# Expert rows loaded in blocks and turned by VectorE, gates loaded apart, and the ends of one expert's second layer placed among the first groups of the next

## The reference

```python
def _attn_ref(r, k, v, w, u):              # 2 x 8 heads x 768 tokens x 48
    for t in range(S):
        cur = np.einsum('bhd,bhe->bhde', u[None] * kt, vt)
        y[:, :, t] = np.einsum('bhd,bhde->bhe', rt, state + cur)
        state = w[None, :, :, None] * state + np.einsum('bhd,bhe->bhde', kt, vt)

def _moe_ref(x, w_in, w_out):              # 1536 x 384, hidden 2048
    h = x @ w_in
    g = np.where(h > 0.0, h, np.exp(np.minimum(h, 0.0)) - 1.0)
    return g @ w_out

def _moe2_ref(x, w_gate, w1, w2, capacity):    # 8 experts, hidden 1024, capacity 384
    expert_idx = np.argmax(x @ w_gate, axis=1)
    gate_w = probs[np.arange(N), expert_idx]   # softmax of the logits
    # tokens go to the slots of their expert in order, up to capacity
    h = np.maximum(np.einsum('ecd,edf->ecf', disp, w1), 0.0)
    y = np.einsum('ecf,efd->ecd', h, w2)
    out[i] = gate_w[i] * y[expert_idx[i], pos[i]]
```

## Time and profile before

| | us |
|---|---|
| median of 3 runs | 415.12 |
| the profiled execution | 415.56 |
| its span | 413.7 |
| granted TensorE clock, mean | 0.997 of full speed (2.4 GHz) |
| PE busy | 406.2 (98% of the span) |
| DVE busy | 242.4 (59%) |
| POOL busy | 231.4 (56%) |
| ACT busy | 188.1 (45%) |

### The profile page before, as it was taken

One profiled execution on the slowest core, in us unless ns is written; L12 is line 12 of the kernel. 1 busy time (PEld: TensorE's weight loads), 2 busy tenths in 40 slices (PEclk: granted clock), 3 DMA queues, 4 the chain that ended last, 5 costly groups with the idle time before them and its releaser, 6 DMA issues.

```text
span 413.7 us, 9445 instructions
## 1 busy us (share of the span) xinstructions
PE 406.2 (98%) x3697; PEld 390.3 (94%) x3697; DVE 242.4 (59%) x576; ACT 188.1 (45%) x409; POOL 231.4 (56%) x239
## 2 busy tenths in 40 slices
PE   8999999999999999999999999999999999999995
PEld 8799799999999999999999999999999999999995
DVE  7787955376576547654663487785635546364522
ACT  4786553233333333333343455552645455474420
POOL 3789865567856685668234336065083562826531
PEclk9999999999999999999999999999999999999998
DMA  7998997214030403020018001827383845729000
GB/s 281 399 395 341 348 371 255 72 49 150 10 119 2 139 21 118 2 87 21 2 19 345 2 2 38 326 77 238 135 304 99 346 147 217 279 100 363 8 31 28
DMA packets 18650, 64.98 MB, mean 157 GB/s; under 512 B 2203, under 2 KB 11717, under 8 KB 16432
## 3 DMA queue, kind: packets, MB, share of 16 engines
q1 hardware_dynamic: 16672, 59.67, 39.5%
q0 software_dynamic: 1792, 4.73, 3.0%
q10 hardware_dynamic: 144, 0.00, 0.0%
HBM read 51.98 MB, written 13.21 MB: 158 GB/s over the span
## 4 chain that ended last, share of the span: by engine, by line
PE 88%; DVE 4%; issue 3%; DMA 3%; POOL 1%; ACT 1%; POOLq 0%; SPq 0%; DVEq 0%
PE bank L1369 26%; PE bank L1371 25%; PE bank L1370 24%; PE bank L1390 2%; DMA xrow<-slots 2%; PE bank L1419 1%; PE bank L1455 1%; PE bank L1459 1%; PE bank L1693 1%; PE bank L1448 1%; PE bank L1451 1%; PE bank L1546 1%; PE bank L1728 1%; PE bank L1729 1%; PE bank L1632 1%
## 5 line engine op out<-in xcount | busy, mean ns | idle before, releaser
L707 POOL TENSOR_TENSOR g_lo<-elu,g_hi 128x256 fp32r<-128x256 f32 x95 | 73.7, 777 | 86.9 <-ACT g_hi L882 86.6
L1369 PE MATMUL bank<-xt,wd_hi 128*128 128x256 f32 x285 | 80.5, 283 | 0.6 <-DVE elu L1197 0.6
L1371 PE MATMUL bank<-xt,wd_lo 128*128 128x256 f32 x285 | 80.4, 282 | 0.0
L1370 PE MATMUL bank<-xt,wd_hi 128*128 128x256 f32 x285 | 80.3, 282 | 0.0
L873 ACT ACTIVATE elu<-elu 128x256 f32<-128x256 f32 x96 | 40.1, 418 | 76.4 <-DVE elu L1189 75.9
L1369 PE MATMUL bank<-wd_hi,g_hi 128*128 128x392 f32 (+1 forms) x192 | 67.4, 351 | 0.0
L1371 PE MATMUL bank<-wd_hi,g_lo 128*128 128x392 f32 (+1 forms) x192 | 65.2, 340 | 0.0
L1370 PE MATMUL bank<-wd_lo,g_hi 128*128 128x392 f32 (+1 forms) x192 | 65.1, 339 | 0.0
L1197 DVE SCALAR_TENSOR_TENSOR elu<-elu,bank 128x256 f32<-128x256 f32 x96 | 40.3, 419 | 41.1 <-ACT elu L873 41.1
L882 ACT CAST g_hi<-elu 128x256 fp32r<-128x256 f32 x96 | 39.0, 406 | 44.1 <-DVE elu L1197 44.1
L1369 PEld LDWEIGHTS bank<-xt,wd_hi 128*128 128x128 f32 x285 | 53.9, 189 | 1.2 <-DVE elu L1197 1.1
(11 more groups left out here) (220 smaller groups left out, 943.7 us busy)
## 6 DMA issues: line engine op xcount, KB each, us to landing
we_raw<-wexp SPq DMA_DIRECT2D x8, 1536.0 KB, 6.5
wd_raw<-wexp SPq DMA_DIRECT2D x8, 1536.0 KB, 7.4
rkt<-rkt SPq DMA_DIRECT2D x12, 512.0 KB, 5.7
nat<-nat SPq DMA_DIRECT2D x9, 672.0 KB, 5.4
xrow<-slots SPq DMA_DIRECT2D x16, 193.0 KB, 7.4
wd_raw<-win SPq DMA_DIRECT2D x4, 768.0 KB, 8.6
wd_raw<-wout SPq DMA_DIRECT2D x4, 768.0 KB, 9.0
wo_tr<-wouttr SPq DMA_DIRECT2D x1, 3072.0 KB, 17.6
```

The costliest lines, as they stand in the source:

```text
L707: nc.gpsimd.tensor_tensor(g_lo[:, f % 4, :], elu[:, f % 2, :], g_hi[:, f % 4, :].bitcast(F32), ALU.subtract).then_inc(s_glo, 1)
L1369: mm(dst, w_hi, x_hi, start=start, stop=False)
L1370: mm(dst, w_hi, x_lo, start=False, stop=False)
L1371: return mm(dst, w_lo, x_hi, start=False, stop=stop)
```

## The change

The rows of experts 1 to 7 come in four transfers instead of two. Transfer p fills 32 partitions with columns 96p to 96p + 95 of all 256 rows, in 8 blocks of 32 rows. DVE turns every 32 x 32 block in one instruction (`expert_cols`), reading every third float, and writes the rows turned into SBUF (`xcol`, on the memory of `x2t`). ACT and DVE split from there, and the six transposes of PE are gone. W1's rows are put in another order on the host (`thirds`) to fit; the places that turn expert 0's rows read every third column (`block_cols`). Gate and token have a transfer and a buffer of their own (`gt`).

SP issues the rows of expert e + 2 as soon as the token numbers of expert e are copied, ahead of its W1; the gates come last. PE's second-layer groups 6 and 7 of an expert stand behind the first-layer groups 0 and 1 of the next, and DVE's output rows behind `ge_lo` of group 1 of the next. `fc2_expert` waits for W2 chunk by chunk, and for each output bank by itself.

In expert 0's second tile, the transposes of the first half stand one first-layer part sooner, those of the second half behind the first group of the second layer. One chunk of expert 1's W1 goes from DVE to POOL, one of its W2 from POOL to DVE.

```diff
             def load_x(e, r):
-                for t in range(2):
-                    sp.dma_start(xrow[r][:, t, :],
-                                 slots[bass.ds(e * CAP + t * 128, 128), :]).then_inc(s_xr[r], 16)
+                for p in range(4):
+                    sp.dma_start(xrow_blocks(r)[32 * p:32 * p + 32, :, :],
+                                 slots[bass.ds(e * CAP, SN), 96 * p:96 * p + 96]
+                                 .rearrange("(b i) c -> i b c", i=32)).then_inc(s_xr[r], 16)
+
+            def load_gt(e, r):
+                sp.dma_start(gt[r][:, :, :], slots[bass.ds(e * CAP, SN), GATE:XR]
+                             .rearrange("(t p) c -> p t c", t=2)).then_inc(s_gt[r], 16)
...
                 for r in range(2):
+                    sp.wait_ge(s_tok[r], i + 1)
+                    load_x(2 * i + 2 + r, r)
                     sp.wait_ge(s_he, ET * (2 * i + r + 1))
                     load_w(2 * i + 2 + r, r)
                     sp.wait_ge(s_fc2e, ET * (2 * i + r + 1))
                     load_w2(2 * i + 2 + r, r)
                     sp.wait_ge(s_ye[r], 2 * (i + 1))
-                    sp.wait_ge(s_tok[r], i + 1)
-                    load_x(2 * i + 2 + r, r)
+                    load_gt(2 * i + 2 + r, r)
...
             def expert_x(i, r):
                 act.wait_ge(s_xtr[r], i + 1)
-                nc.scalar.copy(xe_hi[r][:, 0:2, :], ps_xt[0][:, :].rearrange("p (k n) -> p k n", k=2)).then_inc(s_xehi[r], 1)
-                nc.scalar.copy(xe_hi[r][:, 2, :], ps_xt[1][:, 0:SN]).then_inc(s_xehi[r], 1)
+                nc.scalar.copy(xe_hi[r][:, 0:2, :], xcol[:, 0:2, :]).then_inc(s_xehi[r], 1)
+                nc.scalar.copy(xe_hi[r][:, 2, :], xcol[:, 2, :]).then_inc(s_xehi[r], 1)
...
+            def expert_cols(i, r):
+                dve.wait_ge(s_xr[r], rows_loaded(i, r))
+                V.transpose(xcol.rearrange("p k (b n) -> p b k n", n=32),
+                            xrow_blocks(r).rearrange("p b (n k) -> p b k n", k=KT)).then_inc(s_xtr[r], 1)
...
+                    if f == 1 and behind:
+                        expert_out(bi, br)
...
+                    if more and f == F_X - 1:
+                        expert_cols(ni, nr)
                     if more and f == F_X:
                         expert_x(ni, nr)
                     if f == 5:
-                        dve.wait_ge(s_xr[r], 32 * (i + 1))
+                        dve.wait_ge(s_gt[r], gates_loaded(i, r))
                         wait_if(dve, s_sout[r], 32 * i)
-                        V.tensor_copy(tok_i[r][:, :, :], xrow[r][:, :, TOKEN:XR]).then_inc(s_tok[r], 1)
+                        V.tensor_copy(tok_i[r][:, :, :], gt[r][:, :, 1:2]).then_inc(s_tok[r], 1)
...
+            tile_lo(0, ps_ht[1], s_gehi, s_gelo, ET // 2)
             tile_row(s_he, ET, s_lrow)
-            for b in range(2):
-                tile_lo(b, ps_ht[1], s_gehi, s_gelo, ET // 2)
+            expert_cols(0, 1)
+            tile_lo(1, ps_ht[1], s_gehi, s_gelo, ET // 2)
...
-                    wait_if(pe, s_gelo, q if f == 0 else q - 1)
+                    wait_if(pe, s_gelo, q - 1)
...
                     last.then_inc(s_he, 1)
+                    if f < 2 and behind:
+                        fc2_expert(bi, br, ET - 2 + f)
                     if more and f >= 2:
                         fc2_expert(i, r, f - 2)
...
-                    if more and f == F_X:
-                        expert_x(ni, nr)
-                if more:
-                    fc2_expert(i, r, ET - 2)
-                    fc2_expert(i, r, ET - 1)
```

More of the change, by code:

```diff
@@ L272, in build @@
         s_xr = pair("xrow_loaded")
+        s_gt = pair("gate_and_token_loaded")
         s_xtr = pair("xe_transposed")
@@ L400, in other, with block_cols, xrow_blocks, rows_loaded @@
             return (sems[0], i + 1) if p else (sems[1], i)
+        def block_cols(rows, kt):
+            return rows.rearrange("p (m k) -> p k m", k=KT)[:, kt, :]
+        def xrow_blocks(r):
+            return xrow[r][:, :, :].rearrange("p t c -> p (t c)")[:, 0:2 * DM].rearrange("p (b c) -> p b c", b=8)
+        def rows_loaded(i, r):
+            return NXD * (i + 1) if r else 32 + NXD * i
+        def gates_loaded(i, r):
+            return 16 * (i + 1) if r else 32 + 16 * i
         def wait_if(eng, s, count):
@@ L715, in _, with split_w1_last, split_w2 @@
             pool.wait_ge(s_xr[0], 32)
+            pool.wait_ge(s_gt[0], 32)
             for t in range(BT):
                 scatter_rows(NB - 1, t)
-            def split_w2(e_i, r):
-                for c in range(N1):
+            def split_w1_last():
+                pool.wait_ge(s_ehi[1], N1)
+                cols = slice((N1 - 1) * ECH, N1 * ECH)
+                nc.gpsimd.tensor_tensor(EL[1][:, cols], ER[1][:, cols], EH[1][:, cols].bitcast(F32),
+                                        ALU.subtract).then_inc(s_elo1[1], 1)
+            def split_w2(e_i, r, chunks=N1):
+                for c in range(chunks):
                     pool.wait_ge(s_ehi[r], 2 * N1 * e_i + N1 + c + 1)
@@ L1303, in expert @@
                                            op1=ALU.subtract).then_inc(s_gelo, 1)
+                    if f == 1 and behind:
+                        expert_out(bi, br)
+                    if f == 1 and not behind:
+                        dve.wait_ge(s_ehi[1], 2 * N1)
+                        dve.wait_ge(s_elo2[1], N1 - 1)
+                        cols = slice(W1 + (N1 - 1) * ECH, W1 + N1 * ECH)
+                        V.tensor_tensor(EL[1][:, cols], ER[1][:, cols], EH[1][:, cols].bitcast(F32),
+                                        ALU.subtract).then_inc(s_elo2[1], 1)
                     if more and F_W1 < f <= F_W1 + N1:
@@ L1312, in expert @@
                     if f == 5:
-                        dve.wait_ge(s_xr[r], 32 * (i + 1))
+                        dve.wait_ge(s_gt[r], gates_loaded(i, r))
                         wait_if(dve, s_sout[r], 32 * i)
-                        V.tensor_copy(tok_i[r][:, :, :], xrow[r][:, :, TOKEN:XR]).then_inc(s_tok[r], 1)
[L1316 to L1322, removed]
+                        V.tensor_copy(tok_i[r][:, :, :], gt[r][:, :, 1:2]).then_inc(s_tok[r], 1)
+                if not more:
+                    expert_out(i, r)
+            tile_lo(0, ps_ht[1], s_gehi, s_gelo, ET // 2)
             tile_row(s_he, ET, s_lrow)
-            for b in range(2):
-                tile_lo(b, ps_ht[1], s_gehi, s_gelo, ET // 2)
+            expert_cols(0, 1)
+            tile_lo(1, ps_ht[1], s_gehi, s_gelo, ET // 2)
             expert_x(0, 1)
@@ L1666, in pick_rows @@
                     for t in range(BT):
-                        last = mm(ps_s[0][:, 128 * kt:128 * kt + 128], rows[:, t, NE + 128 * kt:NE + 128 * kt + 128],
+                        last = mm(ps_s[0][:, 128 * kt:128 * kt + 128], block_cols(rows[:, t, NE:NE + DM], kt),
                                   picked[:, t, :], start=False, stop=kt == KT - 1 and t == BT - 1,
@@ L1712, in fc2_expert, with expert @@
                     last.then_inc(s_fc2e, 1)
-            def expert(i, r, more):
+            def expert(i, r, more, behind):
                 ni, nr = (i, 1) if r == 0 else (i + 1, 0)
+                bi, br = (i - 1, 1) if r == 0 else (i, 0)
                 pe.wait_ge(s_elo1[r], N1 * (i + 1) + (0 if r else N1))
@@ L1743, in expert @@
                                 fc2_expert(i, r, f - 2 - t, (t,))
-                    if more and f == F_X:
-                        expert_x(ni, nr)
-                if more:
-                    fc2_expert(i, r, ET - 2)
-                    fc2_expert(i, r, ET - 1)
-                else:
+                if not more:
                     for t in range(2):
@@ L1850 @@
     w_in = moe_w_in[order].reshape(DM // 128, 128, DFF // 128, 128).transpose(1, 2, 0, 3).reshape(128, -1)
+    thirds = [DM // 128 * p + kt for kt in range(DM // 128) for p in range(128)]
     gate_pad = np.zeros((DM, 32), np.float32)
@@ L1867 @@
         "wexp": np.ascontiguousarray(np.stack(
-            [np.concatenate([tiled(moe2_w1[e]), tiled(moe2_w2[e])], axis=1) for e in list(range(NE)) + [0]])),
+            [np.concatenate([tiled(moe2_w1[e][thirds]), tiled(moe2_w2[e])], axis=1) for e in list(range(NE)) + [0]])),
     }
```

99 lines of the change are left out of this document (53 added, 46 removed).

## The result

The changed kernel takes 427.9 us (median of 6 runs, 425.1 to 432.5) against 415.15 for the kernel before on the same chip; the ratio is 1.029 (95% interval 1.026 to 1.032). I had forecast 410.0 with a range of 408.9 to 415.6 and a chance of 0.12 for slower.

What follows compares the result with a forecast made beforehand. PE was taken as the bound, busy 106.01 of 106.10 us. Off came 5.25 (periods) and 0.75 (expert 0's second tile), less 0.85 (a wait in the first turn): 5.15 off 415.12 gives 410.0, range 408.9 to 415.6.

Steps and rivals of the forecast that it cites:

- Transposes off PE and the experts' ends among the next one's groups: Expert 1's start to expert 7's: six periods go from 17.675 to 16.8 us, 5.25 off.
- Expert 0's second tile: Six transposes (0.58 us) leave PE and its two waits become two others: 0.75 off, expert 1 starts at 285.1.
- Strided reads of expert 0's rows: 12 PE operands read with a stride, once: taken as free, under 1 us if loads doubled.
- The ring: Loop from token numbers through W1's issue and landing to the next token numbers: 16.5 us, under PE's 16.8 by 0.3.
- tokens 0.16, all in the earlier trace: DVE's copy of the token numbers, the last part of the loop from W1's landing: 0.16 us.
- slow transpose: Rival: DVE's transpose takes 1.47 us, the loop 17.0, PE waits 0.2 in each of five turns: 411.0; chance 0.15.
- The row transfers themselves: 1024 packets of 384 bytes ahead of W1 in the queue, 22 ns each, 1.4 us per engine: W1 delayed by 0.
- The transpose: DVE's transpose of 768 floats per partition, without a row in the profile: 0.97 us, 0.89 from start to start.
- first turn: Expert 2's W1 waits for the tokens at 284.0, lands at 292.6; PE waits 0.85 us once before expert 1's group 5.
- The gap at an expert's start: Rival: PE's gap at each expert's start stays, only the transposes' time comes: 3.2 off, 411.9; chance 0.10.
- the first wait: PE's single wait before expert 1's group 5, 0.85 us; a rival without it gave 409.1, chance 0.10.
- The slow-queue rival: Row transfers delay W1 by d: loss 6d - 1.5, decisive from packets of 50 ns; 418.1 at 58 ns; chance 0.12.

Runs made afterwards that it cites:

- run 9: Changed kernel with row loads waiting for the transpose that last read their buffer, token numbers behind low part 2, expert 0's columns in the old order: 410.2 us.
- run 10: Run 9 with expert 0's second tile in the order of the kernel before: 410.5 us.
- run 8: Run 5 with expert 0's columns and W1 rows in the order of the kernel before, so PE reads without a stride: 413.0 us.
- run 4: Changed kernel with row loads waiting for the transpose that last read their buffer, instead of for the token numbers: 418.1 us, ratio 1.006.
- run 6: Changed kernel with GpSimd's first W2 chunk waiting for the token numbers of the expert before it: 417.1 us, ratio 1.005.
- run 7: Run 4 with GpSimd's three W2 chunks of 1024 columns cut into six instructions of 512: 411.1 us, ratio 0.990.
- run 3: Changed kernel with W1 issued before the four row transfers, still after the wait for the token numbers: 416.4 us, ratio 1.002.
- run 2: Changed kernel with the rows of experts 1 to 7 loaded as four transfers of 64 whole rows, values not the reference's: 430.9 us, ratio 1.038.
- run 12: Run 9 with VectorE's transposes reading their 768 floats in a row instead of every third, values not the reference's: 410.2 us in one run.
- run 5: Changed kernel with the token numbers made behind VectorE's low part 2 of the same expert instead of low part 5: 415.0 us, ratio 0.999.

## Why the prediction was wrong

*Transposes off PE and the experts' ends among the next one's groups: right.* 6 x 0.875 = 5.25 was the term, and with nothing in the way the period is 16.80 (run 9).

*Expert 0's second tile: size off.* From that stage's first group (275.33 before, 276.63 after) to expert 1's first (285.85 and 286.85) it is 10.52 before and 10.22 after: 0.3 where I had 0.75. The 0.58 of the six transposes brought nothing, since they had filled a wait (run 10); the move brought the 0.3. The wait for a low part stayed, as 0.23.

*Strided reads of expert 0's rows: taken as free, cost 1.08* (run 8). My bound was just too low.

*The ring: the step that failed.* I had seen the ring, and put it at 16.5 against PE's 16.8. It was 20.2, in three terms:
- "tokens 0.16, all in the earlier trace rows". The duration was read from a row at another place in time. There the cast ended 0.2 us before GpSimd started. With the transpose before it, it comes 0.3 after GpSimd's start (in run 4 too, where W1 isn't late), and it took 2.33. With the ring in place it costs about 10 us (run 6); with the ring cut, 7.0 (runs 4 and 7). I listed a slow transpose as a rival and let GpSimd's nearness exclude it; the same neighbour, on the tiny operation behind it, was not among the rivals, although had a row of DVE that I put down to POOL (1955 ns for 1215).
- "The row transfers themselves ... I take 0". ACT starts on W1 after 7.8 in the mean instead of 6.3. In the changed kernel's stretch of 308 to 309 us, 476 packets of 384 bytes took 91.2% of 16 engines, which is 31 ns each; from 309 to 310 it was 35. The line between 16 bytes and a row gave 22, and 50 was the point from which I let it decide. From 309 to 310, behind W1's issue at 308.90, 497 small packets were still served. Of the 1.5 us, 1.1 go with W1 ahead of the rows (run 3); how much of that is the number of packets, run 2 doesn't show, and by my own formula 64 packets of 33 ns would just have been hidden under the issues. The 0.4 left aren't settled; they are in part that I count here to ACT's start, and the earlier trace rows to the landing. The earlier trace rows also held two loads only: the kernel before's last W1 load, issued at 371.19, landed after 7.7.
- The transpose took 1.21 for 0.97, from the stride (run 12). Of these 0.24 only 0.1 shows in the turn, since the other terms of that part were put a little too high (7.8 measured from ACT's start to the cast, 7.7 reckoned).

Together (2.19, 1.47 and 0.07 before rounding) they are 3.7, and 3.7 over 16.5 is the 20.2 measured. In the profiled execution, 432.5, experts 2 to 6 take 99.8 us for 84.0, and expert 1 takes 20.2 where run 7 has 14.9 (2.65 of it PE's wait in the first turn). That is 21.2 of the 21.4 by which it lies above run 7's 411.1. The median, 427.9, is 16.8 above it; no trace shows how the turns of those executions differ.

*The rivals.* The slow transpose was real but small (0.24, not 0.5). The gap at an expert's start is gone (run 9), and the first wait was there. The slow-queue rival had the right formula in its place (a loss in each of five turns, and once more in the first), the wrong cause as the main one, and only 0.12 of the chance. A ring 0.3 us under the pace leaves no room for any error in eight added terms of which two had no row; the range should have gone up to a ring of 18 or more.

*The first turn:* right in kind, 2.04 instead of 0.85 (run 5), from the same late landing (7.9 from 287.56 to 295.43).

## What to carry to other kernels

When a change makes a load wait for something computed from the load before it, write the loop down as a period and compare it with the pace of the bound: if they are within a tenth of each other, forecast by what each term could become, not by what it was. The token numbers, two elements between SBUF and SBUF, had no duration of their own beside GpSimd's chunks: for such an operation look at what GpSimd does at the moment to which the change moves it. The wait on SP should name the last reader of the buffer (`s_xtr`), not a later event that happens to imply it (`s_tok`): that alone gave back 9.8 of the 12.7 us (run 4).

## What the runs showed of the hardware that I had not expected

- VectorE's operation on 2 elements waits for the end of GpSimd's running instruction, as a cast (2.33 us) and as a two-operand maximum (2.32), and half as long when GpSimd's instructions are halved (1.27). Beside GpSimd's scatter it waits too: 0.36, up to the scatter's end.
- Four transfers of 64 whole rows (1544 bytes) took SP 2.49 us to issue, four of 32 partitions with eight pieces of 384 bytes each 1.85.
- PE's six transposes of 128 x 128 took 0.99 instead of 0.67 when their source was read at every third float, and twelve matmuls of that kind 2.10 instead of 1.34.
- VectorE's transpose of 128 x 768 floats took 0.97 us from a contiguous source and 1.21 from every third float.
